# A three-stage routed kernel on one core: a third load buffer, and another order for sums, keys, choice and weight splits

## The reference

```python
# 1: batch 4, heads 8, seq 768, head size 48
for t in range(S):
    cur = u * k_t (outer) v_t
    y_t = r_t @ (state + cur)
    state = w_t[:, None] * state + k_t (outer) v_t
# 2: x is [3072, 384]; 8 experts, hidden 1024
logits = normalize(x) @ normalize(expert_emb).T / tau
e = argmax(logits); gate = softmax(logits)[e]
out = gate * (relu(x @ w1[e]) @ w2[e])
# 3: hidden 2048
h = x @ w_in; g = h * tanh(softplus(h)); out = g @ w_out
```

## Time and profile before

| | us |
|---|---|
| median of 3 runs | 989.7 (980.17, 989.7, 1009.18) |
| the profiled execution | 988.44 |
| its span | 986.4 |
| granted clock of PE at 0.50 (whole stretches of 4 us) | 116 to 124, 184 to 192, 208 to 212, 216 to 236 |
| end of DVE's table (L926) | 225.56 |
| end of PE's matmuls of step 13 (L1101), before `updates(14)` | 176.86 |
| the four operations of `positions(0)` | 179.27 to 180.07 |

### The profile page before, as it was taken

The page is one execution under the profiler, slowest core; times in us unless marked ns, Lnnn a source line. Parts: engine busy times, 40 slices in busy tenths (PEclk is TensorE's granted clock), DMA queues, the critical chain, the costliest instruction groups (busy, mean ns, idle before and its releaser), DMA issues.

```text
span 986.4 us, 17376 instructions
## 1 busy us (share of the span) xinstructions
PE 896.7 (91%) x5639; PEld 791.5 (80%) x5639; DVE 657.0 (67%) x1103; ACT 536.1 (54%) x1059; POOL 466.9 (47%) x273
## 2 busy tenths in 40 slices
PE   2899998845999999999999899999999999999993
PEld 2678787734989898888889688899899889898983
DVE  6888889655364545554634777777777777777772
ACT  2344444222343434343434777787787876877861
POOL 3566755739087266666800322452543632633532
PEclk9999799776999999999999999999999999999996
DMA  7487555544244243345520300100100100100000
GB/s 186 135 242 230 162 155 139 176 141 154 73 160 133 87 168 108 138 137 169 171 72 26 105 1 1 41 24 0 53 11 0 64 0 0 64 0 0 33 1 32
DMA packets 31282, 88.65 MB, mean 90 GB/s; under 512 B 3856, under 2 KB 16112, under 8 KB 31216
## 3 DMA queue, kind: packets, MB, share of 16 engines
q1 hardware_dynamic: 19216, 65.76, 21.9%
q10 hardware_dynamic: 8928, 12.45, 3.8%
q0 software_dynamic: 3072, 9.59, 2.6%
HBM read 70.42 MB, written 17.36 MB: 89 GB/s over the span
## 4 chain that ended last, share of the span: by engine, by line
PE 62%; DVE 8%; issue 5%; ACT 5%; DMA 2%; POOL 1%; another core or an unknown queue 1%; ACTq 0%; DVEq 0%; POOLq 0%
PE ps L1179 14%; PE ps L1180 13%; PE ps L1181 13%; PE ps L1274 6%; PE ps L1275 5%; PE ps L1276 5%; DVE am L1008 3%; PE ps L1205 2%; DMA expert_out<-yo 1%; PE ps L1171 1%; ACT yz L660 1%; ACT yz L657 1%; ACT tn L654 1%; ACT am L640 1%
## 5 line engine op out<-in xcount | busy, mean ns | idle before, releaser
L440 POOL TENSOR_TENSOR gl<-gg,gh 128x512 fp32r<-128x512 f32 x96 | 141.9, 1478 | 300.6 <-DVE gh L1023 294.0
L1274 PE MATMUL ps<-whi,gh 128*128 128x384 f32 x384 | 131.6, 343 | 6.8 <-POOL gl L440 6.4
L1008 DVE SCALAR_TENSOR_TENSOR am<-tn,yz 128x512 f32<-128x512 f32 x96 | 123.9, 1290 | 14.4 <-ACT yz L660 13.4
L1276 PE MATMUL ps<-whi,gl 128*128 128x384 f32 x384 | 130.0, 339 | 0.0
L1275 PE MATMUL ps<-wlo,gh 128*128 128x384 f32 x384 | 130.0, 338 | 0.0
L1013 DVE SCALAR_TENSOR_TENSOR am<-am,yz 128x512 f32<-128x512 f32 x96 | 71.8, 748 | 75.7 <-ACT am L640 75.7
L1179 PE MATMUL ps<-xh,whi 128*128 (+1 forms) x288 | 116.0, 403 | 4.5 <-DVE gg L1019 4.0
L399 POOL TENSOR_TENSOR wlo<-raw,whi 128x1536 fp32r<-128x1536 f32 x32 | 113.2, 3537 | 2.7
L1180 PE MATMUL ps<-xl,whi 128*128 (+1 forms) x288 | 114.2, 396 | 0.0
L1181 PE MATMUL ps<-xh,wlo 128*128 (+1 forms) x288 | 114.1, 396 | 0.0
L640 ACT ACTIVATE am<-am,cst 128x512 f32<-128x512 f32 x96 | 69.4, 723 | 73.1 <-DVE am L1008 73.1
(11 more groups left out here) (154 smaller groups left out, 2033.8 us busy)
## 6 DMA issues: line engine op xcount, KB each, us to landing
raw<-in_wall SPq DMA_DIRECT2D x40, 768.0 KB
rkb<-in_rk SPq DMA_DIRECT2D x16, 672.0 KB, 6.3
xg<-expert_rows ACTq DMA_DIRECT2D x31, 198.0 KB, 2.5
expert_out<-yo ACTq DMA_DIRECT2D x31, 194.0 KB, 3.1
decay<-in_wdec SPq DMA_DIRECT2D x16, 338.6 KB, 3.5
vt_in<-in_vt SPq DMA_DIRECT2D x16, 336.0 KB, 6.8
xin<-expert_out SPq DMA_DIRECT2D x6, 776.0 KB, 4.4
vb<-in_vv SPq DMA_DIRECT2D x16, 288.0 KB, 6.8
```

The costliest lines, as they stand in the source:

```text
L440: nc.gpsimd.tensor_tensor(gl[:, f % 4], gg[:, :], gh[:, f % 4].bitcast(F32), ALU.subtract).then_inc(s_gl, 1)
L1008: nc.vector.scalar_tensor_tensor(out=am[:, par], in0=tn[:, par], scalar=4.0, in1=yz[:, par], op0=ALU.add, op1=ALU.mult).then_inc(s_a, 1)
L1274: pe.matmul(o, high, hi, start=(f == 0), stop=False)
L1276: last = pe.matmul(o, low, hi, start=False, stop=(f == FT2 - 1))
```

## The change

- `rkb` gets a third buffer with a third semaphore; SP loads receptance and keys for step it+4 instead of it+3, and waits for users two steps back instead of one.
- On DVE `outputs(it)` comes before `keys(it+2)`. `positions(0)` comes behind `outputs`, the later `positions(1)` stays ahead of it.
- `choose(0)` is cut in three parts (two, two and three operations), in iterations 9, 10 and 11, at the same place of the iteration.
- ACT makes the first set's high parts in iterations 10, 11, 15, 15. DVE makes the low parts of pieces 0 and 1 in iterations 12 and 13 as before, those of pieces 2 and 3 behind the `link` chain. PE's first `hidden` waits for the first two, its first `project` for all four.

```diff
-    rkb = ar("rkb", [P, 2, 2, S])
+    rkb = ar("rkb", [P, 3, 2, S])
...
-    FIRST_SPLIT = (SLOTS - 4, SLOTS - 3, SLOTS - 2, SLOTS - 2)
+    HIGH_AT = (SLOTS - 6, SLOTS - 5, SLOTS - 1, SLOTS - 1)
+    LOW_AT = (SLOTS - 4, SLOTS - 3)
...
         def load_rk(m):
-            need(sp, s_ks, m - 1)
-            need(sp, s_ra, m - 1)
-            need(sp, s_kr, m - 1)
-            sp.dma_start(rkb[0:ROWS, m % 2], rk[m]).then_inc(s_rk[m % 2], 16)
+            need(sp, s_ks, m - 2)
+            need(sp, s_ra, m - 2)
+            need(sp, s_kr, m - 2)
+            sp.dma_start(rkb[0:ROWS, m % 3], rk[m]).then_inc(s_rk[m % 3], 16)
...
-            if 1 <= it + 3 < SLOTS:
-                load_rk(it + 3)
+            if 1 <= it + 4 < SLOTS:
+                load_rk(it + 4)
...
-            for k in [k for k in range(PIECES) if FIRST_SPLIT[k] == it]:
+            for k in [k for k in range(PIECES) if HIGH_AT[k] == it]:
                 first_high(k)
...
-        def choose(g):
+        def choose(g, parts=(0, 1, 2)):
...
+            if 0 in parts:   # L809, L811
+            if 1 in parts:   # L813, L815
+            if 2 in parts:   # L817, L820, L823
...
-            if it + 2 < SLOTS:
-                keys(it + 2)
-            if it - 2 in CHOOSE_AT:
+            if it - 2 in CHOOSE_AT and it == SLOTS - 1:
                 positions(CHOOSE_AT.index(it - 2))
             if 0 <= it:
                 outputs(it)
+            if it - 2 in CHOOSE_AT and it < SLOTS - 1:
+                positions(CHOOSE_AT.index(it - 2))
+            if it + 2 < SLOTS:
+                keys(it + 2)
...
-            if it in CHOOSE_AT:
+            if CHOOSE_AT[0] - 2 <= it <= CHOOSE_AT[0]:
+                choose(0, (it - CHOOSE_AT[0] + 2,))
+            elif it in CHOOSE_AT:
                 choose(CHOOSE_AT.index(it))
...
-            for k in [k for k in range(PIECES) if FIRST_SPLIT[k] == it]:
+            for k in [k for k in range(PIECES // 2) if LOW_AT[k] == it]:
                 first_low(k)
...
         assert step_of[0] + 1 == R_TAB
+        for k in range(PIECES // 2, PIECES):
+            first_low(k)
...
-            pieces = pe.value_load(tab[0:1, T_WAIT, p:p + 1], min_val=0, max_val=PIECES * E + 2) if p else PIECES + 2
+            pieces = pe.value_load(tab[0:1, T_WAIT, p:p + 1], min_val=0, max_val=PIECES * E + 2) if p else PIECES // 2 + 2
...
         def project(p, at_):
             pe.wait_ge(s_htl, 2 * p + 2)
+            if p == 0:
+                pe.wait_ge(s_lo, PIECES + 2)
```

More of the change, by code:

```diff
@@ L197, in routed_kernel @@
     s_w = [sem("s_w0"), sem("s_w1")]
-    s_rk = [sem("s_rk0"), sem("s_rk1")]
+    s_rk = [sem("s_rk0"), sem("s_rk1"), sem("s_rk2")]
     s_vt = [sem("s_vt0"), sem("s_vt1")]
@@ L371, in receptance @@
         def receptance(m):
-            par = m % 2
             need(pool, s_y, 2 * (m - 2))
-            nc.gpsimd.tensor_tensor(chunks(ra[0:ROWS, m % 3]), chunks(rkb[0:ROWS, par, 0]),
+            nc.gpsimd.tensor_tensor(chunks(ra[0:ROWS, m % 3]), chunks(rkb[0:ROWS, m % 3, 0]),
                                     chunks(pp[0:ROWS, m % 3])[:, :, 0:P], ALU.mult).then_inc(s_ra, 1)
@@ L385, in product_rk @@
             need(pool, s_bon, 2 * (m - 1))
-            nc.gpsimd.tensor_tensor(kr[0:ROWS, par], rkb[0:ROWS, par, 0], rkb[0:ROWS, par, 1], ALU.mult).then_inc(s_kr, 1)
+            nc.gpsimd.tensor_tensor(kr[0:ROWS, par], rkb[0:ROWS, m % 3, 0], rkb[0:ROWS, m % 3, 1], ALU.mult).then_inc(s_kr, 1)
         def scatter(t):
@@ L766, in product @@
             dve.wait_ge(s_seed, m + 1)
-            dve.wait_ge(s_rk[par], 16 * (m // 2 + 1))
+            dve.wait_ge(s_rk[m % 3], 16 * (m // 3 + 1))
             need(dve, s_sc, 3 * (m - 1))
-            nc.vector.tensor_tensor(kb[0:ROWS, par], rkb[0:ROWS, par, 1], seed[0:ROWS, par], ALU.mult).then_inc(s_ks, 1)
+            nc.vector.tensor_tensor(kb[0:ROWS, par], rkb[0:ROWS, m % 3, 1], seed[0:ROWS, par], ALU.mult).then_inc(s_ks, 1)
         def outputs(m):
@@ L806, in choose @@
             sums = C_SUM if n == MOST else C_SUM + (MOST + 1) * E
-            dve.wait_ge(s_lgp, 2 * PAIRS * GROUPS[g][1])
-            need(dve, s_rt, done)
-            nc.vector.tensor_reduce(logit, lgp[:, :, t0:t0 + n].rearrange("p g t e -> p t e g"), AX.X, ALU.add).then_inc(s_rt, 1)
-            dve.wait_ge(s_rt, done + 1)
-            nc.vector.tensor_reduce(top, logit, AX.X, ALU.max).then_inc(s_rt, 1)
-            dve.wait_ge(s_rt, done + 2)
-            nc.vector.tensor_tensor(values_, logit, over_experts(top, n), ALU.is_equal).then_inc(s_rt, 1)
@@ L814, in choose @@
-            dve.wait_ge(s_rt, done + 3)
-            nc.vector.tensor_tensor(values_, values_, over_tiles(rev, n), ALU.mult).then_inc(s_rt, 1)
-            dve.wait_ge(s_rt, done + 4)
-            nc.vector.tensor_reduce(first, values_, AX.X, ALU.max).then_inc(s_rt, 1)
-            dve.wait_ge(s_rt, done + 5)
-            need(dve, s_init, 2)
-            nc.vector.tensor_tensor(by_expert(onehot, g)[:, :, 1:].rearrange("p e t -> p t e"), over_tiles(rev, n),
-                                    over_experts(first, n), ALU.is_equal).then_inc(s_rt, 1)
@@ L822, in choose @@
-            dve.wait_ge(s_rt, done + 6)
-            nc.vector.tensor_tensor_scan(flat(earlier, g), cst[:, sums:sums + (n + 1) * E], flat(onehot, g), 0.0,
-                                         ALU.mult, ALU.add).then_inc(s_rt, 1)
+            if 0 in parts:
+                dve.wait_ge(s_lgp, 2 * PAIRS * GROUPS[g][1])
+                need(dve, s_rt, done)
+                nc.vector.tensor_reduce(logit, lgp[:, :, t0:t0 + n].rearrange("p g t e -> p t e g"), AX.X, ALU.add).then_inc(s_rt, 1)
+                dve.wait_ge(s_rt, done + 1)
+                nc.vector.tensor_reduce(top, logit, AX.X, ALU.max).then_inc(s_rt, 1)
@@ new lines, in choose @@
+            if 1 in parts:
+                dve.wait_ge(s_rt, done + 2)
+                nc.vector.tensor_tensor(values_, logit, over_experts(top, n), ALU.is_equal).then_inc(s_rt, 1)
+                dve.wait_ge(s_rt, done + 3)
+                nc.vector.tensor_tensor(values_, values_, over_tiles(rev, n), ALU.mult).then_inc(s_rt, 1)
+            if 2 in parts:
+                dve.wait_ge(s_rt, done + 4)
+                nc.vector.tensor_reduce(first, values_, AX.X, ALU.max).then_inc(s_rt, 1)
+                dve.wait_ge(s_rt, done + 5)
+                need(dve, s_init, 2)
+                nc.vector.tensor_tensor(by_expert(onehot, g)[:, :, 1:].rearrange("p e t -> p t e"), over_tiles(rev, n),
+                                        over_experts(first, n), ALU.is_equal).then_inc(s_rt, 1)
+                dve.wait_ge(s_rt, done + 6)
+                nc.vector.tensor_tensor_scan(flat(earlier, g), cst[:, sums:sums + (n + 1) * E], flat(onehot, g), 0.0,
+                                             ALU.mult, ALU.add).then_inc(s_rt, 1)
```

## The result

The changed kernel takes 981.9 us in the median, the kernel before 990.1 us in the same series (20 executions each): ratio 0.9936, 95% interval 0.9916 to 0.9957. That is about 6 us by the ratio and 8 us by the medians, where 16.6 us were forecast. The profiled execution takes 982.9 us, its span 980.9 us, 5.5 us less than before's. The time stays within 2% and inside the range of 961 to 983, but the gain is a third to a half of the one forecast.

What follows compares the result with a forecast made beforehand. PE, busy 117.8 of 120 us from 580 us on, was taken as the bound, after a loop of 16 iterations. 988.4 - 6.8 - 7.9 + 1.0 + 0.5 - 2.3 - 2.6 + 1.5 = 971.8 us, range 961 to 983.

Steps and rivals of the forecast that it cites:

- the rest of the kernel moves only as a block: From 580 us on PE is nearly always busy, so only how much earlier its first `hidden` comes matters.
- +1.5: First row load: the second expert's piece 4 is under way beside it, 0 to 2.1 us later, taken as 1.5.
- Third buffer and slow iterations: Loop: waits for loads go, 8.9 us an iteration, 6.8 us gained; two low-clock iterations at full clock, 7.9 gained.
- Sums ahead of keys: DVE in the loop: no work added, PE can't use the gain, taken as 0; 5.5 us kept for a rival.
- The rival in which keys stretch and DVE bounds at 9.4 us: Loop: `keys` behind the sums makes DVE the bound at 9.4 us an iteration, 977 us in all; chance 0.09.
- Thirds: Choice cut over iterations 9 to 11: collisions remain, spread out, 5.0 us against 4.0, so 1.0 us lost.
- Positions and high parts: Iterations 10 to 12: later `rows_out` loses 0.5 us; earlier `positions(0)` lets updates start sooner, 2.3 us gained.
- The second half behind the copies: End of loop: ACT's two high parts come behind `rows_out(14)`, 2.6 us gained; the moved low parts are hidden.
- Slower than before: Iterations 9 to 12: DVE's order and spread choice make PE stand, the clock stays low, 992 us; chance 0.05.
- The scatters: Last row copies: a late low part stops the last scatter, all behind it 1.4 us late, 973 us; chance 0.06.
- the clock holds later too: End of loop: PE's standings shrink to about 1.4 us each, the full clock lasts, 965 us; chance 0.27.

Runs made afterwards that it cites:

- a2: The kernel before with the third buffer and the sums ahead of the keys; ratio to before 0.9928, median -8.6 us.
- a3: The changed kernel with the first choice whole in one iteration again, not in thirds; ratio to before 0.9921, median -9.1 us.
- a4: The changed kernel with all four first pieces split inside the loop, as before; ratio to before 0.9928, median -9.6 us.
- b1: The changed kernel with the third and fourth pieces' loads, high and low parts moved behind the last row copy and first row load; ratio to before 1.0001.
- b2: The changed kernel with `yo`, the weighted rows on their way to memory, in three buffers; ratio to before 0.9958, median -7.9 us.
- b3: The changed kernel with the fifth piece's load held until the first rows have arrived; ratio to before 0.9940, median -9.9 us.
- c3: The kernel before with `yo`, the weighted rows on their way to memory, in three buffers; ratio to before 0.9998, median -0.5 us.
- d4: The kernel before with the row copies held until the last scores are done; ratio to before 0.9991, median -4.4 us.
- c1: The changed kernel with every row copy held until the last positions exist; ratio to before 1.0110, median +9.3 us.
- d1: The changed kernel with the row copies held until the last scores are done; ratio to before 0.9983, median -6.7 us.
- d2: The changed kernel with the row copies held until half of the last outputs are done; ratio to before 1.0022, median -1.0 us.
- b4: The kernel before with the sums ahead of the keys and two buffers still; ratio to before 1.0049, median +0.9 us.
- a1: The kernel before with the third buffer alone, loads two steps back; ratio to before 0.9974, median -4.0 us.
- e1: The changed kernel itself, run once more in another group; ratio to before 0.9933, median -8.2 us.
- c2: The kernel before with only the second half of the first split moved behind the row copies; ratio to before 0.9949, median -4.4 us.
- e2: The changed kernel with the whole first split in the loop and the row copies held until the last scores; ratio to before 0.9900, median -9.1 us.
- d3: The kernel before with third buffer, sums first and the row copies held until the last scores; ratio to before 0.9891, median -13.0 us.
- c4: The changed kernel with every row copy held until the last positions, plus twelve plain copies from SyncE; one execution, 990.75 us.

## Why the prediction was wrong

**The step that failed** is what the prediction had between the loop's full iterations and PE's first `hidden`. It opens with "the rest of the kernel moves only as a block", and for the way there it has five terms (+1.0, +0.5, -2.3, -2.6, +1.5), together 1.9 us shorter; that TensorE, VectorE and ScalarE would stand beside the row copies, and the clock fall behind that, is put at nothing. From the 13th keys to the first L590 the changed kernel took 87.1 us against 81.8, so 5.2 us longer. Of the 14.4 us gained at the 13th keys 9.2 were left there. The expert stage then took 5.4 us more, which is within what one kernel varies (297.7 and 290.6 us for the changed kernel), and the rest 1.7 less, which gives the 5.5 us of this pair.

Other profiles say the same. Eight of kernels with the third buffer, the sums first and copies unheld (a2, a3, a4, b1, b2, b3, the changed kernel twice) have 68.1 to 77.0 us for the stretch, mean 72.8; before, c3 and, with its hold, d4, all three with two buffers and the old order, have 62.8 to 67.6, mean 64.4. The 13th keys come at 135.8 us in the mean of the eight and at 145.7 in the mean of the three. So about 10 us are gained and 8 given back by the profiled executions; the timed ones, of which there are more, keep 6 to 9. What is given back lies behind the 16th keys, 37.3 against 27.1 us to the last positions; ahead of them the eight are 2 us shorter. With the copies away it isn't given back: from the 16th keys to the last positions the changed kernel then takes 19.0 to 19.1 us (c1, d1, d2), where the eight have 32.9 to 38.7. The kernel before takes 25.2 with d1's hold (d4), and 30.6 and 25.5 without (before, c3), so its copies cost it far less.

**Third buffer and slow iterations**, -6.8 and -7.9: close in their sum for this pair of executions (14.4 measured against 14.7, 1.0 of the 14.4 already there at the third keys), and by luck, since the parts are off. The stable part is that an iteration takes 9.0 us on average. The 7.9 us for the lost clock were one execution's; c3's loop has no such fall, and only 8.4 us lie between its 13th keys and those of the changed kernel. Nor does DVE's wait for the load show as what set PE's pace. From b4's waits between 20 and 135 us:

```profile
DVE kb L769 <- issue: 12.8, 8, 2.8
```

b4 has two buffers and these 12.8 us of waits, and still 9.2 us an iteration between the 3rd and the 13th keys. c3, also with the waits, has 9.8; a1, with the buffer and without them, 9.9, of which 0.3 are for the one iteration at a low clock.

**Sums ahead of keys**, 0: mis-sized. In the loop the order is worth more than the buffer, as b4 and a1 show, each by one profile. In the time the buffer alone has -4.0 us, with the sums -8.6, and the sums alone are worth nothing (b4, +0.9). I had read the 8.8 us of PE's shortest iteration as what is next late; with keys ahead it is every second one only. The rival in which keys stretch and DVE bounds at 9.4 us didn't come.

**Thirds**, +1.0: 33.1 us for the three iterations against 31.6, so 1.5, with the low clock of this execution in it. Where the clock held, the thirds took 31.9 to 32.0 us (a4, b2, b3, c1, d1, e1), and a2 without them 30.3: 1.7. a3 without them is no faster in time.

**Positions and high parts**, -2.3 and +0.5: updates wait 1.47 us instead of 3.36, the iteration is 14.1 us instead of 15.3, so -1.2.

**The second half behind the copies**, -2.6: ACT's high parts are out of the way as said, but no gain shows in the stretch. c2, this move alone, is the one sign of it. The reason that the low parts are hidden held (POOL's splits end at 241.0 and PE isn't late), but they release weight loads beside the first row load. I had priced that at 1.5, and the first rows came 1.9 us later behind the positions. With the copies held (d1) the same loads met the copies, and the last one landed 3.5 us later than in a2.

**The rivals.** "Slower than before" had the right mechanism, new standing of PE, then a clock that stays low, with the wrong origin; I put it on DVE's order in iterations 9 to 12 and gave it 0.05. In e1 the clock is at 0.50 from 175.3 to 199.2 us, and PE's stop beside the fifth copy runs from 171.6 to 173.5. The scatters weren't held up by the low parts. That the clock holds later too is what c1 and d1 show once the copies are away: 53.2 us at 1.00.

**What stays open.** What of GpSimd's copies stops the others. In all nine profiles with the sums first and copies unheld (the eight and b4) PE's first stop begins 5.3 us after the first copy, at the start of the fifth. In a1 the first stop is ScalarE's, 6 us after it, in before also (the only long one next to the copies, 8.75 us), 9 us after it, and in e2 again ScalarE's, 0.7 us after it. DVE's low part of 1.76 us runs within 1.5 us of that moment in all of these but a1, and in d1, where no low part meets the first copies, there is no stop. But in c2, c3, d3 and d4 a low part meets copies and nothing stops, in d4 the very first copy, as in e2. I have no run that tells which meeting it takes. Nor is it shown why two buffers with the old order suffer less: there the first copy starts 5.2 to 5.6 us ahead of the last keys, with the sums first 3.3 us (b4 with two buffers too). That this decides was only argued, and a1 with 6.3 us and a stretch of 74.5 speaks against it.

## What to carry to other kernels

A gain in a steady loop reaches the end only if the stretch behind it doesn't change its company: ask what now runs beside what, and price the clock with every new stop of TensorE: in e1 it cost more than the standing (11.2 against 6.7 us). A move that is "hidden" has to be followed through what it releases: the low parts cost nothing, the loads that waited for them cost 1.9 us in the changed kernel and 3.5 us on a copy's landing in d1. Where executions spread by 1 to 2%, no stage of a single profile is a property of the kernel; the loop of the 14 profiles with buffer and sums agreed within 3 us (13th keys at 134.6 to 137.2), the expert stage of the changed kernel alone varied by 7.

## What the runs showed of the hardware

- Twelve plain copies from SyncE of 194 KB each didn't stop TensorE (c4, one execution). Beside scattered ones of about the same size from GpSimd TensorE stood for 1.1 to 8.0 us (the changed kernel, a1) with no visible releaser, ScalarE up to 8.8 (before) and VectorE up to 7.4 us (the changed kernel, waits for the stopped TensorE among them), with matmuls coming in fours at 0.75 us gaps. In d1 twelve scattered copies did none of this.
- An indirect copy takes 0.97 us to prepare. One that began while a VectorE subtraction of 128x1536 (1.76 us) was running took 1.36 us where half a microsecond overlapped (the changed kernel) and 2.35 us where 1.5 us did (before); one that began just ahead of it kept its 0.97 (the changed kernel's last).
- With two 768 KB loads released 5.0 and 3.3 us before the last scattered copy was prepared, it landed 5.3 us after that (d1), otherwise 1.6 to 1.9 us after it.
- A VectorE step of 128x8 elements took 3.50 us where a GpSimd subtraction of 3.52 us ran; the shortest of the kernel's 31 took 0.22 and the middle one 0.69. From the changed kernel:

```profile
446.81 3.52 POOL L399 TENSOR_TENSOR wlo<-raw,whi 128x1536 fp32r<-128x1536 f32 x1
446.85 3.50 DVE L953 TENSOR_SCALAR shifted<-xg,gs 128x8 f32<-128x8 f32 x1
```
